# Rebuilding the start of a fused attention and MoE kernel, and spreading its early weight splits

## The reference

```python
q_bits = (q @ proj > 0); k_bits = (k @ proj > 0)        # six bits each
mask   = q_bucket[:, :, :, None] == k_bucket[:, :, None, :]
scores = where(mask, q @ k.T / sqrt(64), -1e9)
attn   = exp(scores - max) / (sum + 1e-9)
x      = attn @ v                                        # then heads side by side: 1536 x 512
x      = (sigmoid(x @ w_gate) * (x @ w_val)) @ w_out     # 512 -> 1536 -> 512
h      = x @ w_in                                        # 512 -> 2048
g      = where(h >= 1, h, where(h <= -1, 0, (h + 1)**2 / 4))
out    = g @ w_out2
```

## Time and profile before

| | |
|---|---|
| median of three runs | 849.15 us (848.2 to 850.33) |
| the profiled execution's own time | 852.1 us |
| its span | 850.3 us |
| PE busy in the span | 806.6 us (95%) |
| DVE, ACT, POOL busy | 374.4, 395.8, 239.8 us |
| share of the chain that ended last | PE 78%, DVE 5%, SPq 5%, POOL 5%, ACT 4% |

### The profile page before, as it was taken

One profiled execution on the slowest core, in us unless ns is written; L12 is line 12 of the kernel. 1 busy time (PEld: TensorE's weight loads), 2 busy tenths in 40 slices (PEclk: granted clock), 3 DMA queues, 4 the chain that ended last, 5 costly groups with the idle time before them and its releaser, 6 DMA issues.

```text
span 850.3 us, 10601 instructions
## 1 busy us (share of the span) xinstructions
PE 806.6 (95%) x3984; PEld 687.7 (81%) x3984; DVE 374.4 (44%) x615; ACT 395.8 (47%) x642; POOL 239.8 (28%) x242
## 2 busy tenths in 40 slices
PE   3679999999998989999999999999999999999998
PEld 3578788899897878888888888888888888888886
DVE  2367778887787331113111311114433443344333
ACT  1368788898898633312111222334533443344332
POOL 0245776665668574300000003442200000000000
PEclk9599999999999999999999999999999999999999
DMA  4977447538430043200000003230000100010001
GB/s 98 227 134 159 106 86 156 123 75 171 113 100 1 1 150 111 87 1 1 0 1 1 1 0 99 76 124 26 25 1 1 50 1 1 1 49 1 1 1 49
DMA packets 62978, 51.15 MB, mean 60 GB/s; under 512 B 29008, under 2 KB 52304, under 8 KB 62800
## 3 DMA queue, kind: packets, MB, share of 16 engines
q1 hardware_dynamic: 62928, 50.48, 24.3%
HBM read 27.27 MB, written 3.15 MB: 36 GB/s over the span
## 4 chain that ended last, share of the span: by engine, by line
PE 78%; DVE 5%; SPq 5%; POOL 5%; ACT 4%; issue 2%; DMA 1%; POOLq 0%; ACTq 0%
PE ps L524 16%; PE ps L526 16%; PE ps L525 16%; PE ps L637 5%; PE ps L639 5%; PE ps L638 5%; PE ps L504 4%; PE ps L492 3%; PE ps L495 2%; PE ps L517 2%; PE ps L518 2%; SPq L265 2%; DVE probs L878 2%; POOL probs L399 1%; SPq L296 1%
## 5 line engine op out<-in xcount | busy, mean ns | idle before, releaser
L524 PE MATMUL ps<-xh,arena 128*128 128x512 f32 x480 | 186.9, 389 | 0.0
L526 PE MATMUL ps<-xh,arena 128*128 128x512 f32 x480 | 186.8, 389 | 0.0
L525 PE MATMUL ps<-xl,arena 128*128 128x512 f32 x480 | 186.8, 389 | 0.0
L407 POOL TENSOR_TENSOR arena<-stage,arena 128x1024 fp32r<-128x1024 f32 (+2 forms) x32 | 81.3, 2548 | 244.1 <-ACT arena L698 243.9
L927 DVE TENSOR_TENSOR gate<-ps,gate 128x512 f32<-128x512 f32 x36 | 24.9, 691 | 205.3 <-ACT gate L749 205.3
L889 DVE TENSOR_TENSOR body<-ps,body 128x768 fp32r<-128x768 f32 x96 | 91.3, 951 | 37.4 <-ACT body L675 37.0
L524 PEld LDWEIGHTS ps<-xh,arena 128*128 128x128 f32 x480 | 90.1, 188 | 18.8 <-issue 0.2
L525 PEld LDWEIGHTS ps<-xl,arena 128*128 128x128 f32 x480 | 90.1, 188 | 18.7
L526 PEld LDWEIGHTS ps<-xh,arena 128*128 128x128 f32 x480 | 90.1, 188 | 18.7
L878 DVE TENSOR_SCALAR_CACHE_REDUCE probs<-ps 128x768 f32<-128x768 f32 x96 | 91.3, 951 | 28.5 <-PE ps L495 26.1
L679 ACT ACTIVATE probs<-probs,small 128x768 f32<-128x768 f32 x96 | 90.1, 939 | 28.8 <-DVE probs L878 28.6
(11 more groups left out here) (81 smaller groups left out, 1169.2 us busy)
## 6 DMA issues: line engine op xcount, KB each, us to landing
stage<-in_moe_w_out_dram SPq DMA_DIRECT2D x28, 256.0 KB, 3.3
body<-qh SPq DMA_DIRECT2D x32, 192.0 KB
body<-kh SPq DMA_DIRECT2D x32, 192.0 KB
stage<-in_moe_w_in_dram SPq DMA_DIRECT2D x16, 256.0 KB, 2.8
qn<-in_q_dram SPq DMA_DIRECT2D x16, 192.0 KB, 4.3
kn<-in_k_dram SPq DMA_DIRECT2D x16, 192.0 KB, 5.5
body<-ql SPq DMA_DIRECT2D x16, 192.0 KB
body<-kl SPq DMA_DIRECT2D x16, 192.0 KB
```

Of the source, the lines that this page charges most:

```text
L524: pe.matmul(dst, wh, ah, start=start, stop=False)
L525: pe.matmul(dst, wh, al, start=False, stop=False)
L526: return pe.matmul(dst, wl, ah, start=False, stop=stop)
```

## The change

It rebuilds the start of the program and moves some work of the attention stage:

- K of pair 0 is loaded on ScalarE's DMA queue while SyncE loads Q. V of heads 0 and 1 is loaded before the first copies.
- The tensor engine transposes the identity matrix 14 times before the first turn, 6 times after the turns and 12 times after the signs, into a PSUM slot that is written later anyway (`keep_busy`).
- `q1` and `q2` of a head lie side by side, and one DMA writes the high part of Q into both. ScalarE's queue issues the two copies of K's high part for head 0.
- For head 0 the codes take no DMA: VectorE writes the Q codes from PSUM into `q2`, ScalarE the scaled K codes from `bits` into `k2`.
- The semaphore `placed` becomes `copied` (five DMAs a head) and `coded` (four). What waits to overwrite the turned Q waits for the copies alone, and what overwrites `codes` for the codes alone.
- In pair 0 the turns, high and low parts, signs, bits and scaled codes of pair 1 come two steps later (`late`).
- SyncE's order for pair 0 becomes: Q, projection, both V, head 0's copies, head 1's copies, Q and K of pair 1, head 1's codes, weights.
- The six early weight parts are spread: one in each of pairs 1 to 6, on ScalarE at u = 6 and on GpSimd at u = 8.

The diff, cut to its core:

```diff
+        def late(i):
+            return 0 if i else 2
...
-            if g % U < 2 and g // U < NP - 1:
-                uses.append(("QK"[g % U], g // U + 1))
+            if late(g // U) <= g % U < late(g // U) + 2 and g // U < NP - 1:
+                uses.append(("QK"[g % U - late(g // U)], g // U + 1))
...
-                    copy_rows(i, xx, q1[p][xx][0:D, :], qh)
-                    copy_rows(i, xx, q2[p][xx][0:D, :], qh)
+                    src = qh[D * xx:D * xx + D, :].rearrange("p (w n) -> p w n", w=1)
+                    sp.dma_start(qs[p][xx][0:D].bitcast(F32),
+                                 src.bitcast(F32).to_broadcast([D, 2, S])).then_inc(copied[p][xx], 16)
...
             load_q(0)
-            load_k(0)
             sp.dma_start(projn[0:D, :], proj).then_inc(proj_in, 16)
             sp.dma_start(projn[D:P, :], proj).then_inc(proj_in, 16)
+            load_v(0)
+            load_v(1)
             place_q(0, (0,))
             place_k(0, (0,))
-            place_codes(0, (0,))
+            place_q(0, (1,))
+            place_k(0, (1,))
             load_q(1)
             load_k(1)
-            load_v(0)
-            place_q(0, (1,))
-            place_k(0, (1,))
             place_codes(0, (1,))
-            load_v(1)
             stage1(0, 0)
             stage1(1, 1)
...
-                if i in (1, 2) and 7 <= u < 10:
-                    low_w(i - 1, C1, 2 * C1 * (i - 1), (u - 7,), 3)
+                if 1 <= i < 7 and u == 8:
+                    low_w((i - 1) // 3, C1, 2 * C1 * ((i - 1) // 3), ((i - 1) % 3,), 3)
...
+            def keep_busy(n):
+                idle = score_slot(0)
+                for _ in range(n):
+                    pe.transpose(idle[:, 0, 0:P], ident[:, :], ident[:, :])
+            keep_busy(14)
             turn("Q", 0)
             turn("K", 0)
+            keep_busy(6)
             pe.wait_ge(setup, 3)
             signs(0, False)
             signs(0, True)
+            keep_busy(12)
...
-                if u == 3 and i < NP - 1:
+                if u == late(i) + 3 and i < NP - 1:
                     signs(i + 1, False)
...
+            for xx in range(2):
+                act.dma_start(kn[:, :, xx, :], kv[xx]).then_inc(k_in, 16)
             high_turned("Q", 0)
             high_turned("K", 0)
+            act.wait_ge(k_high, 1)
+            for rows in (slice(0, D), slice(D, P)):
+                act.dma_start(k1[0][0][rows, :].bitcast(F32), kh[0:D, :].bitcast(F32)).then_inc(copied[0][0], 16)
+            act.wait_ge(z_bits, 1)
+            for c in (2, 3):
+                act.activation(k2[0][0][D:D + MR, G * (c % 2):G * (c % 2) + G], bits[32 * c:32 * c + MR, :], ACT.Copy,
+                               scale=-MASK).then_inc(first_k_codes, 1)
...
-                if i in (1, 2) and 4 <= u < 7:
-                    high_w(i - 1, (u - 4,), 3)
+                if 1 <= i < 7 and u == 6:
+                    high_w((i - 1) // 3, ((i - 1) % 3,), 3)
...
             make_bits(0)
+            for c in range(2):
+                rows = slice(32 * c, 32 * c + MR)
+                dve.tensor_scalar(q2[0][0][D:D + MR, G * c:G * c + G], z_bank[rows, :], 0.0, code[rows, :], ALU.is_gt,
+                                  ALU.add).then_inc(first_q_codes, 1)
```

More of the change, by code:

```diff
@@ L96, in carve @@
             return body[:, at[0] - n:at[0]]
-        q1 = [[carve(S) for _ in range(2)] for _ in range(2)]
-        q2 = [[carve(S) for _ in range(2)] for _ in range(2)]
+        qs = [[carve(2 * S).rearrange("p (w n) -> p w n", w=2) for _ in range(2)] for _ in range(2)]
+        q1 = [[both[:, 0, :] for both in heads] for heads in qs]
+        q2 = [[both[:, 1, :] for both in heads] for heads in qs]
         k1 = [[carve(S) for _ in range(2)] for _ in range(2)]
@@ L206, in freed, with all_copied, all_coded @@
             return ends[last], m + 1
[L208 to L209 removed]
+        def all_copied(i):
+            return 16 * 5 * (i // 2 + 1)
+        def all_coded(i, xx):
+            return 16 * 4 * (i // 2 + 1 - (i % 2 == 0 and xx == 0))
         w_staged = [sem(f"w_staged{i}") for i in range(2)]
[L212 removed]
+        w_high, high_parts, w_split = sem("w_high"), sem("high_parts"), sem("w_split")
         xh_ready, xl_ready = sem("xh_ready"), sem("xl_ready")
@@ L295, in place_codes @@
                         row = 32 * c + MR * xx
-                        sp.dma_start(dst.bitcast(F32), codes[row:row + MR, :]).then_inc(placed[p][xx], 16)
+                        sp.dma_start(dst.bitcast(F32), codes[row:row + MR, :]).then_inc(coded[p][xx], 16)
             def stage1(f, slot):
@@ L402, in low_w @@
             def low_w(f, width, off, parts=(0,), of=1):
-                pool.wait_ge(w_high, f + 1)
+                if of - 1 in parts:
+                    pool.wait_ge(w_high, f + 1)
+                else:
+                    pool.wait_ge(high_parts, (of - 1) * f + parts[-1] + 1)
                 for i in parts:
@@ L563, in _ @@
                     weigh(j, part)
-                if u == 0 and i < NP - 1:
+                if u == late(i) and i < NP - 1:
                     turn("Q", i + 1)
-                if u == 1 and i < NP - 1:
+                if u == late(i) + 1 and i < NP - 1:
                     turn("K", i + 1)
@@ L698, in high_w @@
                     last = act.copy(arena[:, off + a:off + b], staged(f % 2, a, b))
+                    if of > 1 and i < of - 1:
+                        last.then_inc(high_parts, 1)
                 if of - 1 in parts:
                     last.then_inc(w_high, 1)
+            for xx in range(2):
+                act.dma_start(kn[:, :, xx, :], kv[xx]).then_inc(k_in, 16)
             high_turned("Q", 0)
             high_turned("K", 0)
+            act.wait_ge(k_high, 1)
+            for rows in (slice(0, D), slice(D, P)):
+                act.dma_start(k1[0][0][rows, :].bitcast(F32), kh[0:D, :].bitcast(F32)).then_inc(copied[0][0], 16)
[3 more added lines that the diff above has]
+                               scale=-MASK).then_inc(first_k_codes, 1)
             for g in range(STEPS):
                 i, u = g // U, g % U
-                if u == 1 and i < NP - 1:
+                if u == late(i) + 1 and i < NP - 1:
                     high_turned("Q", i + 1)
-                if u == 2 and i < NP - 1:
+                if u == late(i) + 2 and i < NP - 1:
                     high_turned("K", i + 1)
@@ L912, in _ @@
                     low_probs(g - LAG)
-                if u == 4 and i < NP - 1:
+                if u == late(i) + 4 and i < NP - 1:
                     make_bits(i + 1)
```

51 lines of the change are left out of this document (31 added, 20 removed).

## The result

The changed kernel takes 844.67 us (median of 15 runs, 840.91 to 847.49) against 850.13 us (15 runs, 847.48 to 853.98): ratio 0.9931, 95% interval 0.9914 to 0.9948, a gain of 5.9 us by that ratio, with 4.4 to 7.3 as its interval (the medians lie 5.5 us apart). The forecast was a gain of 11.1 us and a time of 838.0 us; the measured time lies just above the range of 832 to 844.

The account below looks back on a forecast made before the run. It took the start to be bound by SyncE's DMA issues and the DMA engines up to step 12; gains of 9.4 us there and 1.7 from the weight parts, 11.1 in all, take the 849.15 us median to 838.0; range 832 to 844.

Parts of the forecast that it names:

- What this is worth at step 12: Start, SyncE's issues and DMA bytes summed up to the second pair's first scores: 49.3 us, a gain of 9.4 us.
- No new hole: Check on pair 1's later turn: high Q ready at 24, SyncE there at 24.6, so the queue would not stand idle.
- step 12: Second pair's first scores on the tensor engine, at 58.69 us before; its date was the number to predict, 49.3.
- The sum's 48.3: Sum of SyncE's issues: 32.8 us of issuing from 10.3 until 43.1, plus 5.2 us to the codes' landing.
- The parts: Six weight parts spread over six attention pairs: 0.3 us cost a pair, a gain of 1.7 us.
- (a) Loads: Start, first loads on two queues: Q at 5.5, K at 5.8, Q's low part starting at 8.4 us.
- (b) Filler: Filler transposes in the tensor engine's early waits: cost nothing; at 2.4 GHz signs take 2.1 us instead of 4.1.
- (c) Codes in place: Head 0's codes written by VectorE and ScalarE without DMA: 1.2 us of writes, in place at 13.5 us.
- (d) Copies of head 0: Head 0's copies, 1.18 MB, end near 14.6, later than the codes; first scores at 14.6 us instead of 20.73.
- The later turn: Pair 1's turn two steps later: tensor engine waits some 5 us for Q, step 6 at 30.5, no harm.
- The second rival: Part of the start's gain lost to lagging DMA engines or late Q: step 12 at 53.5, 843 us; chance 0.19.
- The first rival: Tensor engine's own chain, not DMA, sets step 12: 45.2, gain 13.5, 834.0 us; chance 0.22.

Follow-up runs that it names:

- e2: Changed kernel with head 1's four code DMAs issued on ScalarE's queue instead of SyncE's; one profiled execution, span 837.7 us against 843.4.
- e1: Changed kernel with its six early weight loads moved behind pair 1's codes and V loads; 840.74 us, ratio 0.9893 to the kernel before.
- f2: Kernel before the change, unchanged, profiled a fourth time; span 847.6 us against 850.3 in its first profile.
- e12: Changed kernel with K's load and the two copies of K's high part back on SyncE's queue; one profiled execution, span 842.2 us.
- e4: Changed kernel without its 32 filler transposes of the identity; one profiled execution, 847.8 us.
- e8: Changed kernel with late weights, head 1's codes on ScalarE, pair 1's Q/K loads before head 1's copies, weight parts in steps 4 and 5; 837.59 us, ratio 0.9846.

## Why the prediction was wrong

The step that failed is **"What this is worth at step 12", with its check "No new hole"**. I let SP reach pair 1's copies at 24.6; it reached them at 29.06. Of these 4.5 us, 1.05 came in at the start (K's low copy issued at 11.35 instead of 10.3), 0.4 with that copy (0.97 for 0.6), and the 13.7 us for what lies between became 16.7 from 12.32 to 29.02. I had priced copies at the 0.6 us that an issue takes on an unsaturated queue, while I counted the engines as saturated from 8.5 us on; both can't be. In the saturated stretch the issues took what their bytes take (1.97 MB from 12.32 to 22.25 are 198 GB/s, the stretch as a whole moved 209), so SP could not gain a lead: it finished the loads at 22.25, the engines at 24.6, 2.4 us later, and the four codes that followed took 3.5 us. The hole that I had seen at 15.6 us in the kernel before was not removed but moved to 24.6. e2 closes it alone and gets step 12 to 48.39.

That hole is not all of it. My check "No new hole" also had Q's high part ready at 24; it was ready at 26.45 here, and in e1 and e2, where nothing else held the queue, the first copy waited for it until 26.7. So with the codes out of the way 2.1 of the 4.5 us would still have been lost; what made up for it in e2 is the stretch behind, 21.7 us instead of my 23.7. The sum's 48.3 comes out right in e2 by two errors that cancel.

In size: step 12 came at 51.8 in the mean of four profiles (52.8 in the first) instead of 49.3, 2.5 us. The parts gave 1.2 instead of 1.7. That leaves about 2 us of the 5.2 us shortfall, and where they went stays open. They are not in the dates: the kernel before has step 12 at 58.6 in the mean of its five profiles, as in the first (58.69). A candidate is the base. The first profiled execution stood 2.95 us above the median and I treated its chain as typical; the five together took 852.6 us in the mean, 2.5 us above the median of the 15 runs, and the four of the changed kernel 843.9, 0.8 us below theirs, so the profiles show a gain of 8.7 us where the runs show 5.5 to 5.9. Only f2 was near the median (849.36 us), with step 12 at 57.48, K's turn at 63.17 and no drop of the clock. That the unprofiled runs look like f2, so that less was to be won from there, is argued from their times, not shown.

Point by point:
- (a) Loads: Q landed for 6.6, not 5.5 (5.96 to 7.0 over the kernels with two queues; 5.5 in e12 with one, which fits two loads sharing the engines). The low part of Q started at 9.50, before at 9.68, where I had 8.4: the projection landed at 6.97, 3.85 us after its second issue and not 2.9. Small, but it is the 1 us by which the rest was late.
- (b) Filler: free, as forecast. The signs took 2.4 us (10.60 to the bits at 12.96) instead of 4.1. Whether that bought anything at step 12 is what e4 left open.
- (c) Codes in place: the two writes took 1.25 us on DVE and 1.06 on ACT, forecast 1.2, and were there at 14.9.
- (d) Copies of head 0 end last, as forecast: PE's wait at 16.56 is put down to K's low copy. 16.56 instead of 14.6, since that copy went out at 11.35 and not at 10.3 and was there 5.2 us later and not 4.3.
- The later turn: PE waited 5.12 us for pair 1's Q (forecast 5), which came at 24.06 instead of 22, step 6 at 35.8 instead of 30.5: the low parts came later, and the granted clock was 0.51 (1.2 GHz) from 22 to 36 us, for which I had no term. It was hidden behind the queue: PE was ready at 48.95, 3.75 us after my 45.2, and waited.
- The second rival, part of the gain lost, is what happened, with step 12 at 51.8 rather than 53.5; its reason "SP finds Q not ready" did not in the changed kernel (it waited for nothing there), only in e1 and e2, for 0.8 and 0.5 us. The first rival, that PE's chain decides, is what e1 and e8 show once the queue is relieved, at 48.4 to 48.8 instead of 45.2.

## What to carry to other kernels

When one in-order queue feeds a stage, lay its issues out against the engines' backlog: small DMAs hide only behind a lead, and here the queue was only some 2.4 us ahead of the saturated engines. Take what is not needed yet (here 1.57 MB of weights) out of the stretch before the date that counts: two lines moved on top of the rebuild brought the gain from 5.9 to 9.0 us. Whether they alone would have given as much in the kernel before was not run. And profile the kernel before more than once: a forecast built on the chain of one execution that lies off the median may count on time that most runs do not lose.

## What the runs showed that I had not expected

- One DMA that writes 384 KB inside SBUF takes 0.68 us to issue on a free queue (at 8.37 us) and 1.91 us while the engines are saturated (at 12.32 us).
- The 14 transposes end by 4.8 us in every run, yet Q's turn ran at 2.4 GHz (0.88 us) in five of the twelve runs with filler and at 1.2 GHz (1.54 us) in seven. The signs behind it ran at 2.4 GHz in the changed kernel's first profile and in its third, one of each kind.
- Four code DMAs of 18 KB took 3.5 us to issue, longer than six weight loads of 256 KB (3.2 us).
